# Attention scores of two steps side by side, on one core

## The reference

```python
for e in range(E):                       # 4 experts, 64 wide
    scores = scale * (q @ k.T)           # causal: later keys get -1e9
    a = np.exp(scores - scores.max(-1, keepdims=True))
    a /= a.sum(-1, keepdims=True) + 1e-09
    ye = a @ v @ wo[e]
    out += gate[e] * ye                  # gate: softmax over the two best of x @ w_gate
```

## Time and profile before

| | |
|---|---|
| time, median of 3 runs (lowest to highest) | 694.41 us (693.5 to 694.41) |
| the profiled execution's own time | 694.48 us |
| its span, first to last instruction | 692.7 us |
| granted TensorE clock | 1.000 of 2.4 GHz |
| PE busy | 675.4 us (98%) |
| DVE, ACT, POOL busy | 401.7 (58%), 322.1 (46%), 152.6 (22%) us |
| chain that ended last | PE 87%, DVE 7%, ACT 3%, issue 2% |

### The profile page before, as it was taken

The page is one execution under the profiler, slowest core; times in us unless marked ns, Lnnn a source line. Parts: engine busy times, 40 slices in busy tenths (PEclk is TensorE's granted clock), DMA queues, the critical chain, the costliest instruction groups (busy, mean ns, idle before and its releaser), DMA issues.

```text
span 692.7 us, 12293 instructions
## 1 busy us (share of the span) xinstructions
PE 675.4 (98%) x4784; PEld 444.0 (64%) x4784; DVE 401.7 (58%) x795; ACT 322.1 (46%) x805; POOL 152.6 (22%) x200
## 2 busy tenths in 40 slices
PE   7998999999999999999999999999999999999998
PEld 7876656676656665676656665676665666566554
DVE  6999986392865567546574828747377223661200
ACT  2456656423661266722655136662276314563340
POOL 7663610061202520017010522005320000000000
PEclk9999999999999999999999999999999999999999
DMA  9998400005300180000700053000000000000000
GB/s 225 298 352 231 154 0 1 1 12 144 115 1 1 44 225 2 1 1 25 245 2 0 2 143 126 1 1 2 35 0 2 1 25 12 0 1 12 23 1 34
DMA packets 36921, 43.35 MB, mean 63 GB/s; under 512 B 2560, under 2 KB 27264, under 8 KB 36608
## 3 DMA queue, kind: packets, MB, share of 16 engines
q1 hardware_dynamic: 36864, 42.57, 21.0%
HBM read 37.84 MB, written 4.72 MB: 61 GB/s over the span
## 4 chain that ended last, share of the span: by engine, by line
PE 87%; DVE 7%; ACT 3%; issue 2%; POOL 1%; DVEq 0%; POOLq 0%; ACTq 0%
PE bank L951 76%; PE bank L955 6%; PE bank L1117 3%; PE bank L1113 2%; DVE nmax L707 2%; ACT shared L459 1%; DVE shared L720 1%; DVE idec L673 1%; DVE bank L700 1%; ACT L540 1%; DVE att L740 0%; ACT shared L468 0%; DVE rinv L717 0%; POOL rk_sb L355 0%; DVE rinv L715 0%
## 5 line engine op out<-in xcount | busy, mean ns | idle before, releaser
L951 PE MATMUL bank<-wv_sb,k_sb 128*128 128x384 f32 x384 | 139.4, 497 | 0.0
L951 PE MATMUL bank<-xk_sb,wk_sb 128*128 128x384 f32 x384 | 138.6, 500 | 0.6 <-ACT act_sb L443 0.6
L951 PEld LDWEIGHTS bank<-xk_sb,wk_sb 128*128 128x128 f32 x384 | 68.4, 189 | 50.2 <-issue 8.5
L951 PEld LDWEIGHTS bank<-wv_sb,k_sb 128*128 128x128 f32 x384 | 67.5, 190 | 38.8 <-issue 3.7
L459 ACT ACTIVATE shared<-bank,nmax 128x128 f32<-128x128 f32 (+5 forms) x96 | 59.9, 629 | 56.4 <-DVE nmax L707 56.3
L673 DVE RECIPROCAL idec<-dec 112x260 f32<-112x260 f32 x48 | 82.8, 1754 | 0.6
L386 POOL TENSOR_TENSOR state<-state,carry 112x512 f32<-112x512 f32 x20 | 22.0, 1099 | 252.4 <-DVE state L759 133.3
L951 PE MATMUL bank<-xT_sb,wqk_sb 128*128 128x384 f32 (+1 forms) x240 | 64.1, 424 | 0.6 <-ACT xT_sb L515 0.6
L497 ACT ACTIVATE att<-ident,bonus 128x128 f32<-128x128 f32 x192 | 58.1, 392 | 10.9 <-DVE bonus L681 10.9
L694 DVE TENSOR_TENSOR out_sb<-bank,sg_sb 128x384 f32<-128x384 f32 x24 | 13.3, 556 | 85.2 <-PE bank L951 85.0
L515 ACT COPY xT_sb<-bank 128x384 f32<-128x384 f32 x24 | 11.5, 480 | 98.3 <-PE bank L1117 98.3
(11 more groups left out here) (93 smaller groups left out, 927.7 us busy)
## 6 DMA issues: line engine op xcount, KB each, us to landing
rk_sb<-in_rk SPq DMA_DIRECT2D x24, 384.0 KB, 6.9
v_sb<-in_v SPq DMA_DIRECT2D x24, 256.0 KB, 7.4
w_sb<-in_wT SPq DMA_DIRECT2D x24, 227.5 KB, 5.0
r_sb<-in_rT SPq DMA_DIRECT2D x24, 224.0 KB, 5.5
k_sb<-in_kT SPq DMA_DIRECT2D x24, 224.0 KB, 6.1
out<-out_sb SPq DMA_DIRECT2D x24, 192.0 KB, 1.9
wk_sb<-in_w_k SPq DMA_DIRECT2D x1, 1536.0 KB, 10.8
wv_sb<-in_w_v SPq DMA_DIRECT2D x1, 1536.0 KB, 15.2
```

Of the source, the lines that this page charges most:

```text
L951: return nc.tensor.matmul(out, lhsT, rhs, start=start, stop=stop)
```

## The change

In words:

- `attention_step` of PE: `fill_a(0)` is empty, and `fill_a(1)` holds groups 0 and 1. So scores of step 0 and of step 1 stand in a row, and then both fill groups.
- Group 1 is computed in bank 6 instead of 7. It waits for `r_ready` instead of the relu of group 0, and the first output waits for the relu of group 1. The third block of `mix_gate` of all halves goes to bank 6 instead of 3, and waits for the eviction of the first values instead of the first keys. Scores of step 1 wait for nothing any more.
- DVE takes the maxima of steps 0 and 1, then computes the gates, then scales.
- ACT computes the exponentials of steps 0 and 1, then relu 0 and relu 1.
- In steps 0 and 1 of odd halves PE adds the mask by matmul, and DVE leaves out its copy_predicated.

The diff:

```diff
--- before.py
+++ after.py
@@ -84,17 +84,17 @@
 def mix_bank(hh, i):
 
     if i < FT and hh != LAST:
-        return 7
+        return 6 if i == 1 else 7
     return RING[i % 3] if hh == LAST else RING[i - FT]
 
 
 def r_bank(h, t):
-    return (4, 5, 6 if h == LAST else 3)[t]
+    return (4, 5, 6)[t]
 
 
 def fill_a(i):
 
-    groups = {0: ((0,), ()), 1: ((1,), ()), 2: ((), (2,)), 3: ((), (3,)), 4: ((), (4,)), 5: ((), (5,)), 6: ((6,), (7,))}[i]
+    groups = {0: ((), ()), 1: ((0, 1), ()), 2: ((), (2,)), 3: ((), (3,)), 4: ((), (4,)), 5: ((), (5,)), 6: ((6,), (7,))}[i]
     return tuple([q for g in place for q in range(KT * g, KT * (g + 1))] for place in groups)
 
 
@@ -219,6 +219,14 @@
                 lo = 2 * (i % 2) + e
                 return bank[:, lo, :]
             return bank[:, 2 * e:2 * e + 2, :].rearrange("p a x -> p (a x)")
+
+        def masked_by_pe(h, i):
+
+            return h == 0 or (h % 2 == 1 and i < QM)
+
+        def masked_until(h, i):
+
+            return sum(not masked_by_pe(a, x) for a in range(h + 1) for x in range(STEPS if a < h else i + 1))
 
         def diagonal_blocks(h, i):
 
@@ -475,8 +483,10 @@
             def attention_step(h, i):
                 if i < STEPS:
                     exponentials(h, i)
-                    relu(h - 1, i)
+                    if i == 1:
+                        relu(h - 1, 0)
                     if i >= 1:
+                        relu(h - 1, i)
                         transposed(h, i - 1)
                         square(h - 1, i - 1)
                 else:
@@ -695,15 +705,15 @@
 
             def maxima(h, i):
                 w = width(h, i)
-                if h > 0:
+                if not masked_by_pe(h, i):
                     dve.wait_ge(score_psum, h * TILES + 2 * i + 2)
                     d.copy_predicated(diagonal_blocks(h, i), bc(before[:, :].bitcast(mybir.dt.int32).unsqueeze(1), [P, 2, P]),
                                       bc(masked_out[:, :].unsqueeze(1), [P, 2, P])).then_inc(score_masked, 1)
-                    dve.wait_ge(score_masked, (h - 1) * STEPS + i + 1)
+                    dve.wait_ge(score_masked, masked_until(h, i))
                 for e in range(2):
                     n = 2 * i + e
-                    if h == 0:
-                        dve.wait_ge(score_psum, n + 1)
+                    if masked_by_pe(h, i):
+                        dve.wait_ge(score_psum, h * TILES + n + 1)
                     d.tensor_reduce(nmax[:, n:n + 1], scores(h, i, e)[:, 0:w], axis=AX.X, op=ALU.max, negate=True).then_inc(max_ready, 1)
 
             def scale(h, m):
@@ -724,7 +734,10 @@
             def attention_step(h, i):
                 if 1 <= i <= STEPS:
                     scale(h, i - 1)
-                if i < STEPS:
+                if i == 0:
+                    maxima(h, 0)
+                    maxima(h, 1)
+                elif 2 <= i < STEPS:
                     maxima(h, i)
                 if 2 <= i < STEPS + 2:
                     m = i - 2
@@ -964,8 +977,10 @@
                         pe.wait_ge(*((relu_ready, hh * FT + i - 2) if i - 3 < FT else (out_ready, hh * HC + i - 2 - FT)))
                     elif hh == LAST:
                         pe.wait_ge(out_ready, (hh - 1) * HC + i + 1)
+                    elif hidden and i == 1:
+                        pe.wait_ge(r_ready, (hh + 1) * HC)
                     elif hidden and i > 0:
-                        pe.wait_ge(relu_ready, hh * FT + i)
+                        pe.wait_ge(relu_ready, hh * FT + (i if i > 2 else 1))
                     elif hidden and hh > 0:
                         pe.wait_ge(out_ready, (hh - 1) * HC + 1)
                     elif i == FT:
@@ -1003,17 +1018,15 @@
                     pe.wait_ge(prob_ready, h * TILES + 2 * i)
                 elif i >= 2:
                     pe.wait_ge(prob_ready, h * TILES + 2 * i - 2)
-                if i == 1 and h > 0:
-                    pe.wait_ge(r_ready, h * HC)
                 for lo in range(0, w, 512):
                     hi = min(w, lo + 512)
                     for e in range(2):
                         rows = slice(HD * e, HD * e + HD)
                         x = mm(scores(h, i, e)[:, lo:hi], qk_sb[rows, m, q0:w], qk_sb[rows, QM + m, lo:hi],
-                               stop=h > 0 or hi != w)
-                        if h > 0 and hi == w:
+                               stop=not masked_by_pe(h, i) or hi != w)
+                        if not masked_by_pe(h, i) and hi == w:
                             x.then_inc(score_psum, 1)
-                for e in range(2 if h == 0 else 0):
+                for e in range(2 if masked_by_pe(h, i) else 0):
                     mm(scores(h, i, e)[:, q0:w], ident_b[:, :], later_b[:, :], start=False).then_inc(score_psum, 1)
 
             def output(h, m):
@@ -1024,6 +1037,8 @@
                     pe.wait_ge(oT_ready, h * STEPS + m)
                 elif h == 0:
                     pe.wait_ge(ktok_ready, NC - 1)
+                else:
+                    pe.wait_ge(relu_ready, (h - 1) * FT + 2)
                 for j in range(qt + 1):
                     for e in range(2):
                         x = 2 * (m % QM) + e
@@ -1207,7 +1222,7 @@
                     if c == 1 and h < LAST:
                         pe.wait_ge(proj_act, h * QM + 1)
                     if c == 2 and h < LAST:
-                        pe.wait_ge(proj_dve, h * (QM + HC) + 1)
+                        pe.wait_ge(proj_dve, h * (QM + HC) + QM + 1)
                     for t in range(KT):
                         i = mm(bank[:, r_bank(h, c), 0:F], xr_sb[:, t, c * P:(c + 1) * P], wr_sb[:, t, :],
                                start=t == 0, stop=t == KT - 1)
```

## The result

The changed kernel takes 688.56 us (median of 4 runs, 687.9 to 689.09), the kernel before on the same chip 693.95 (692.93 to 694.41). The ratio is 0.9925, 95% interval 0.9912 to 0.9937: 5.4 us less. I had forecast 690.0 with a range of 688.8 to 693.0.

A forecast was written before the change was run, and what follows sets the result against it. PE, busy 98% of the span, was taken as the bound. Gains of 2.4 us (even halves), 1.5 (three odd halves) and 0.6 (h = 1) sum to 4.5, from 694.48 to 690.0 us; range 688.8 to 693.0.

The forecast's parts named there:

- The gain of h = 1: First odd half, where PE waited 0.99 instead of 0.60 us: between 0.5 and 0.9 us less, 0.6 taken.
- The place and the views: The whole gain lies in the first two attention steps of seven halves, h = 1 to 7, seen in PE's waits and timelines.
- Even halves: h = 2, 4, 6, start of step 0's scores to first output: 0.85 us less worked out, 0.8 taken, 2.4 in three.
- the ties on ScalarE and VectorE: Even halves: ScalarE's copy due at 5.55 us plus 0.05 against PE's 5.59; VectorE's probabilities at 4.3 to 4.65 against 4.57.
- Odd halves, 3, 5, 7: Start of step 0's scores to step 2's scores: 7.95 us becomes 7.43; 0.5 taken each, 1.5 in three.
- The mask pair behind step 1: Odd halves, PE's second pair of mask matmuls, with full matmuls behind it: charged 0.20 us.
- VectorE's tie: Odd halves, step 0's transposes: scaled probabilities ready 6.47 us after step 0's scores start, needed by PE at 6.46.
- (1): Rival: moved work makes a new wait in odd or even halves, so half the gain comes back; 692 us, chance 0.14.
- (2): Rival: PE arrives earlier at later steps and linear attention but waits there for VectorE or GpSimd; 694.3 us, chance 0.08.
- (3): Rival: VectorE becomes the bound at step 0's transposes, each reduction taking twice 0.645 us; 700.5 us, chance 0.04.
- The cost of a change between narrow and full matmuls: Tiling-mode changes drain PE: even halves go from four changes to two, odd halves keep four; trace agrees by 0.17 us.
- The price of a pair by formula: Skill's issue gap gives 0.11 us per mask pair, eight pairs 0.9 instead of 1.7 us; the trace's 0.22 was preferred.

The follow-up runs named there:

- masks first: Changed kernel with an odd half's four mask matmuls ahead of step 0's scores, scores added in pieces of 384 and 128 columns: 688.28 us, ratio 0.9921.
- Masks alone: Kernel before with only the masks of steps 0 and 1 of odd halves moved to PE; order, banks and waits kept: 691.02 us, ratio 0.9953.
- order alone: Changed kernel with VectorE's masks kept in all steps of halves 1 to 7: 690.83 us, ratio 0.995.
- masks twice: Changed kernel with each mask matmul of odd halves issued twice: 689.04 us, ratio 0.9939.
- odd halves only: Against the kernel before, new order and masks by PE in h = 1, 3, 5, 7 alone, old order in even halves: 690.8 us, ratio 0.995.
- second profile of the changed kernel: Changed kernel run once more, unaltered, on the same chip as three other variants: 688.86 us, ratio 0.9923 to the kernel before.

## Why the prediction came out as it did

- **The steps that failed** are two terms of the sum. The gain of h = 1 was mis-sized (0.6 taken, 1.05 measured; the other six halves add 0.40 together), and the gain was subtracted from one execution of 694.48 us, where the median beside the changed kernel was 693.95. I had written that the spread of the base does not matter here. The range of 688.8 to 693.0 stands for a gain of 1.5 to 5.7 us from 694.48, and the measured 5.4 lies in it. So the time fell below the range by the two misses together; with either of them put right the range would have held it.
- **The place and the views** were right: every microsecond was won between T0 and the first output of seven halves.
- **Even halves.** Working: 0.85 each. Measured 0.84 to 0.85. The close hit has some luck in it: the twelve fill instructions took 0.05 more than worked out, and I had taken the ties on ScalarE and VectorE as just covered. I took 0.8 for no reason but caution, which cost 0.13 us over three.
- **Odd halves, 3, 5, 7.** I took 0.5 each, and measured were 0.47, 0.65, 0.65. Two sizes were off. The mask pair behind step 1 was charged 0.20 and took 0.12; and I ended the sum at step 2's scores, where the output behind them came another 0.06 us earlier, because ScalarE's copy no longer held it up (it ended 0.05 us ahead of the output before, at 270.09 in h = 3, and 0.54 ahead now, at 431.17 in h = 5). VectorE's tie (ready at T0 + 6.47, needed at 6.46 by my sum) was real, but both came earlier. In h = 5 its first reduction starts at T0 + 1.33 and not 1.42, the scaled probabilities end at T0 + 6.29, and PE starts the transposes at 6.39. What is left of slack is less than the 0.22 us of the delay in h = 3, which makes PE 0.13 us late, and less than the 0.2 us that masks first wins and loses again. Together 0.27 us.
- **h = 1, the largest miss: 0.6 taken, 1.05 measured.** I saw 0.39 us more wait there and let it pass to the new order in large part, as a late VectorE. VectorE had been late (0.65 us between two instructions that are 0.27 apart in h = 3), but by a delay that sits at one place in the instruction stream. The changed stream has it elsewhere. That it went is luck of the new stream and no merit of the change. In h = 3, where 0.23 us of delay now stand, the first output comes 0.18 later (8.82 against the 8.64 without it). By that the 0.38 us of before would cost some 0.33 in h = 1, an estimate. The miss is 0.45 us.
- **The sum.** 4.5 + 0.13 + 0.27 + 0.45 = 5.35, as measured from the timelines. The other 0.5 us between forecast and median is the base: I subtracted from one execution of 694.48 us, and the median beside the changed kernel was 693.95.
- **The range** failed on its lower end. The bounds that I had worked out reached 687.8, and I cut them to 688.8 as unlikely, without adding that the base itself varies by half a microsecond.
- **The reason given for the odd halves was half wrong.** I credited the new order and the masks together. Masks alone give 8.69, order alone 9.32, both 8.65. There the order brings 0.05 us where no delay takes it back. So in the odd halves the forecast was near for a reason that was in part not the one at work.
- **Rivals.** Nothing came back but the 0.13 us of h = 3 (1), nothing was lost later (2, the 80.08 and 70.80 us), and four reductions took 2.57 us, 0.64 each (3).
- **The cost of a change between narrow and full matmuls.** A pair of masks took 0.22 us between scores, 0.12 ahead of full matmuls and 0.11 where it adds no change. So adding a change costs about 0.1, and moving one adds nothing. The rule of the Trainium skill that changing the tiling mode drains the engine (TensorEngine Tiling (Array Packing), Key Properties) agrees with these prices. They do not prove it: score matmuls take half as long per column as full ones (0.056 against 0.109 us for 128 columns, from the working above), and no run separates a drain from what a short run of scores loses at its ends.
- **The price of a pair by formula.** The gap for one warm matmul in the Trainium skill (TensorE: Matmul & The Clock Gate, Back-to-back issue gap) gives an estimate of 0.11 us for a pair, and masks twice measured that. As the price at its place it was half of the 0.22 between scores, and near the 0.12 ahead of full matmuls, where I had charged 0.20.

## What to carry to other kernels

Where the bounding engine waits for a chain over others, taking one short step off the chain can pay even if the bounding engine has to do it itself; ask what it costs at that place, next to which neighbours. A wait is worth only what the wait behind it leaves, so removed waits are to be followed to the next fixed point (here the first output), and a new order, its buffers and the work of the other engines are tried apart as well as together. A sum made against one execution needs the spread of the base in its range.

## What the runs showed of the hardware

- The kernel opens with 72 matmuls of 128 columns that keep PE busy. Their total time differs between executions. The kernel before, and below its timeline the stretches 8 to 9 and 12 to 13 us (length, PE's busy time with the number of its instructions, granted clock, DMA share, GB/s):

```profile
4.00 11.22 PE L951 MATMUL bank<-ident 128*128 128x128 f32 x72 [4.00 <-POOL tri L344]
15.15 1.16 PE L951 MATMUL bank<-r_sb,k_sb 48*128 48x128 f32 x16
...
8.00:9.00 1.00, 1.00 (x6) 1.00 1.20 237
12.00:13.00 1.00, 1.00 (x11) 1.00 1.06 232
```

The kernel with odd halves only, with its stretch from 8 to 9 us:

```profile
3.99 9.76 PE L969 MATMUL bank<-ident 128*128 128x128 f32 x72 [3.99 <-POOL tri L357]
13.68 1.16 PE L969 MATMUL bank<-r_sb,k_sb 48*128 48x128 f32 x16
...
8.00:9.00 1.00, 1.00 (x11) 1.00 1.21 249
```

In all thirteen traces the 72 matmuls go at 6 or 7 per microsecond first and at 11 or 12 from some moment on (counted with those that reach over an edge). That moment lies in the eighth microsecond with odd halves only and in the tenth or eleventh in the kernel before. The granted clock reads 1.00 (of 2.4 GHz) in both stretches, so this column does not show what changes the rate. The first real matmul then starts between 13.68 and 15.15 us, and all that follows is shifted.
- In twelve traces h = 1's T0 follows the first real matmul 78.6 to 78.7 us later; in the second profile of the changed kernel it was 79.5. There PE waited for a DMA, and the first profile has no such wait:

```profile
23.90 2.92 PE L964 MATMUL bank<-xT_sb,wqk_sb 128*128 128x128 f32 x24 [0.59 <-DMA wvg_sb<-in_wvg]
```

Behind that T0 the two profiles differ by 0.01 us over 495.6. So the 1.4 us between them arise in the first half batch: 0.6 in the 72 matmuls and 0.8 behind them, up to h = 1.
- A delay of 0.23 to 0.48 us on VectorE came and went, or moved, with the number of instructions ahead of it. An effect of that size in one of several like places is no evidence of what the work costs.
